# Row sums two steps earlier, four score buffers, and bias and head copies moved between engines

## What is computed

```python
# attention: each query sees the 8 first keys and the last 96
scores = scale * q @ k.T + (-slope[h] * dist)      # masked outside the window
scores = scores - max(scores)
a = exp(scores)
a = a / (sum(a) + 1e-9)
x = a @ v                                          # (1536, 512)
# first feed forward, 512 -> 2048 -> 512
h = x @ w_in
g = (a0 + a1*h + a2*h**2 + a3*h**3) / (1 + |b0|*|h| + |b1|*h**2 + 1e-6)
x = g @ w_out
# second, 512 -> 1024 -> 512
h = x @ w2_in
s = h * softmax(h)
out = layer_norm(s) * g_ln @ w2_out
```

## Time and profile before

| | |
|---|---|
| median of 3 runs | 487.11 us (486.02 to 490.15) |
| the profiled execution | 483.23 us, of which its span 481.2 us |
| PE busy | 469.0 us (97%) |
| DVE busy | 377.9 us (79%) |
| ACT busy | 271.3 us (56%) |
| POOL busy | 55.8 us (12%) |
| granted TensorE clock | 1.00 throughout |

### The profile page before, as it was taken

One profiled execution on the slowest core, in us unless ns is written; L12 is line 12 of the kernel. 1 busy time (PEld: TensorE's weight loads), 2 busy tenths in 40 slices (PEclk: granted clock), 3 DMA queues, 4 the chain that ended last, 5 costly groups with the idle time before them and its releaser, 6 DMA issues.

```text
span 481.2 us, 7546 instructions
## 1 busy us (share of the span) xinstructions
PE 469.0 (97%) x2734; PEld 383.1 (80%) x2734; DVE 377.9 (79%) x705; ACT 271.3 (56%) x481; POOL 55.8 (12%) x123
## 2 busy tenths in 40 slices
PE   7889999999999999999999999999999999999997
PEld 5667778888888878888888788888888888888885
DVE  6989989999999989877889999999685555555550
ACT  6989998656656465455555545543454333333341
POOL 4868770000000000000000000000000000000000
PEclk9999999999999999999999999999999999999999
DMA  8897964000000000000033445331012222222201
GB/s 296 295 384 268 350 252 178 1 0 1 0 1 1 0 1 0 1 1 0 1 93 105 131 140 158 113 93 44 1 44 67 66 65 65 65 68 78 72 23 44
DMA packets 25665, 42.91 MB, mean 89 GB/s; under 512 B 2080, under 2 KB 16800, under 8 KB 24480
## 3 DMA queue, kind: packets, MB, share of 16 engines
q1 hardware_dynamic: 23760, 36.64, 22.2%
q0 software_dynamic: 1296, 5.24, 3.7%
q10 hardware_dynamic: 576, 0.60, 0.4%
HBM read 33.04 MB, written 3.15 MB: 75 GB/s over the span
## 4 chain that ended last, share of the span: by engine, by line
PE 85%; ACT 7%; DMA 3%; DVE 3%; POOL 1%; issue 1%; SPq 0%; ACTq 0%; DVEq 0%
PE ps L1198 9%; PE ps L1199 9%; PE ps L1200 9%; PE ps L1129 8%; PE ps L1130 8%; PE ps L1131 8%; ACT probs L481 5%; PE ps L1263 5%; PE ps L1261 5%; PE ps L1218 5%; PE ps L1262 5%; PE ps L1217 5%; PE ps L1216 5%; PE ps L1244 2%; DMA bank_a_raw<-in_w_in 2%; PE ps L1095 2%
## 5 line engine op out<-in xcount | busy, mean ns | idle before, releaser
L1198 PE MATMUL ps<-gate_hi,bank_b_hi 128*128 128x512 f32 x192 | 74.9, 390 | 0.5 <-DVE tok_lo L942 0.5
L1129 PE MATMUL ps<-tok_hi,bank_a_hi 128*128 128x512 f32 x192 | 75.1, 391 | 0.0
L1130 PE MATMUL ps<-tok_lo,bank_a_hi 128*128 128x512 f32 x192 | 74.7, 389 | 0.0
L1199 PE MATMUL ps<-gate_lo,bank_b_hi 128*128 128x512 f32 x192 | 74.7, 389 | 0.0
L1131 PE MATMUL ps<-tok_hi,bank_a_lo 128*128 128x512 f32 x192 | 74.7, 389 | 0.0
L1200 PE MATMUL ps<-gate_hi,bank_b_lo 128*128 128x512 f32 x192 | 74.7, 389 | 0.0
L543 ACT ACTIVATE quad<-ps 128x1024 f32<-128x1024 f32 x23 | 23.7, 1030 | 57.8 <-DVE rest L880 57.8
L481 ACT ACTIVATE probs<-negs,small 128x256 f32<-128x256 f32 (+1 forms) x96 | 46.0, 484 | 0.8 <-DVE small L726 0.7
L442 POOL TENSOR_SCALAR probs<-probs,small 128x256 f32<-128x256 f32 (+1 forms) x96 | 42.6, 465 | 15.4 <-DVE small L737 15.4
L862 DVE SCALAR_TENSOR_TENSOR quad<-quad,small,absh 128x1024 f32<-128x1024 f32 x23 | 29.5, 1281 | 18.0 <-ACT absh L546 17.8
L1198 PEld LDWEIGHTS ps<-gate_hi,bank_b_hi 128*128 128x128 f32 x192 | 36.0, 188 | 8.7 <-issue 1.2
(11 more groups left out here) (103 smaller groups left out, 948.1 us busy)
## 6 DMA issues: line engine op xcount, KB each, us to landing
v_sb<-in_v_win SPq DMA_DIRECT2D x8, 704.0 KB, 6.6
bank_a_raw<-in_w_in SPq DMA_DIRECT2D x4, 1024.0 KB, 9.0
bank_b_raw<-in_w_out SPq DMA_DIRECT2D x4, 1024.0 KB, 7.1
stage_hi<-tok_hi SPq DMA_DIRECT2D x12, 256.0 KB, 2.7
stage_lo<-tok_lo SPq DMA_DIRECT2D x12, 256.0 KB, 2.8
out_dram<-out_sb SPq DMA_DIRECT2D x12, 256.0 KB, 2.0
q_sb<-in_q_t SPq DMA_DIRECT2D x14, 192.0 KB, 5.1
k_sb<-in_k_win SPq DMA_DIRECT2D x7, 384.0 KB, 8.2
```

What stands on the lines that cost most here:

```text
L1129: pe.matmul(banks(bank, 1), bank_a_hi[:, f, ws], x_hi, start=(k == 0), stop=False)
L1130: pe.matmul(banks(bank, 1), bank_a_hi[:, f, ws], x_lo, start=False, stop=False)
L1198: pe.matmul(banks(4 + k, 1), bank_b_hi[:, f, ws], g_hi, start=first, stop=False)
L1199: pe.matmul(banks(4 + k, 1), bank_b_hi[:, f, ws], g_lo, start=False, stop=False)
```

## The change

Seven things are changed, all in the attention:

1. `SUMS_AHEAD` is 4: step n makes the sums and reciprocals of units n+4 and n+5. They also stand later in the step, behind the copy of the transposed half.
2. There are four `negs` buffers. The two new ones lie in free room and in the end of `tok_hi` and `tok_lo`, which is written last.
3. The biases of the pairs of heads 1 to 3 are made by POOL (`next_bias`), behind the units 1, 3, 5 and 7 of the twelve before, and have two buffers in turn. DVE makes only the first one (`attend_bias(h)`).
4. Four of the sixteen copies to `tok_hi`, those of m = 5, 14, 23 and 32, go from ACT to DVE (`attend_high`), in front of the low part in the steps 8, 18, 26 and 36.
5. POOL's low parts of `w_in` stand behind the units 21, 23, 33 and 35 in place of 15, 21, 27 and 33.
6. POOL issues the cast of `w_in` behind unit 7 in place of 8.
7. Two waits of PE for `heads_hi`, which the wait for `heads_lo` includes, are gone.

```diff
-    negs = [[at(f"negs{i}{h}", [P, WIN], F32, w + (2 * i + h) * KB) for h in range(2)] for i in range(2)]
+    NB_NEGS = 4
...
+    bias_odd = [at(f"bias_odd{h}", [P, NB], F32, (TOK_HI, TOK_LO)[h] + 4 * (KT * T - NB)) for h in range(2)]
+    biases = (bias, bias_odd)
...
-    AHEAD, SCORES_AHEAD, SUMS_AHEAD = 6, 8, 2
+    AHEAD, SCORES_AHEAD, SUMS_AHEAD = 6, 8, 4
...
-    POOL_IN, SPLIT_FROM, SPLIT_EVERY = 4, 15, 6
-    LOADS_AT, CAST_AT = (1, 3, 4, 5), 8
+    POOL_IN, SPLITS_AT = 4, (21, 23, 33, 35)
+    LOADS_AT, CAST_AT = (1, 3, 4, 5), 7
...
+    HIGH_ON_DVE = (5, 14, 23, 32)
...
+        def next_bias(pr, h, cols):
+            pool.tensor_scalar(biases[pr % 2][h][:, cols], dist[:, cols], small[:, SLOPE_COL + 2 * pr + h:SLOPE_COL + 2 * pr + h + 1],
+                               1.0, ALU.mult, ALU.mult).then_inc(pool_bias, 1)
+
+        BIAS_AT = {1: (0, slice(WIN, NB)), 3: (1, slice(WIN, NB)), 5: (0, slice(0, WIN)), 7: (1, slice(0, WIN))}
...
-                f, part = divmod(n - SPLIT_FROM, SPLIT_EVERY)
-                if part == 0 and 0 <= f < POOL_IN:
-                    split_in_low(f)
+                if n % NPB in BIAS_AT and n // NPB + 1 < PAIRS:
+                    next_bias(n // NPB + 1, *BIAS_AT[n % NPB])
+                if n in SPLITS_AT:
+                    split_in_low(SPLITS_AT.index(n))
...
             for m in outs_at(n):
-                attend_out(m)
+                if m not in HIGH_ON_DVE:
+                    attend_out(m)
...
-            if h == 0 and n >= 2:
-                dve.wait_ge(exp_ready, 2 * (n - 1))
+            if h == 0 and n >= NB_NEGS:
+                dve.wait_ge(exp_ready, 2 * (n - NB_NEGS + 1))
...
+        def attend_high(n):
...
+            dve.wait_ge(values_ready, n + 1)
+            dve.tensor_copy(tok_hi[:].rearrange("p k t -> p (k t)")[:, bass.ds(pr * T + (b * S + half * HALF), HALF)],
+                            banks(6 + half, 1, HALF)).then_inc(high_dve, 1)
...
-            if n + SUMS_AHEAD < HEADS:
-                attend_sums(n + SUMS_AHEAD)
             if k < HEADS:
                 if pr and m == 0:
-                    dve.wait_ge(bias_ready, 4 * pr)
+                    dve.wait_ge(pool_bias, 4 * pr - 2)
                 attend_shift(k, 0)
-                if pr and m == 0:
-                    dve.wait_ge(shifted_ready, 2 * k)
-                    attend_bias(pr, 0, OF_WINDOW)
-            if n + SUMS_AHEAD < HEADS:
-                attend_reciprocals(n + SUMS_AHEAD)
             if k < HEADS:
                 attend_shift(k, 1)
...
             attend_copy(n)
...
+            if n + SUMS_AHEAD < HEADS:
+                attend_sums(n + SUMS_AHEAD)
             if k < HEADS:
-                for h in range(2):
-                    attend_shift(k + 1, h)
-            if k < HEADS and m == BLOCKS + 2 and pr + 1 < PAIRS:
-                for h in range(2):
-                    attend_bias(pr + 1, h, OF_FIRST)
+                if pr and m == 0:
+                    dve.wait_ge(pool_bias, 4 * pr)
+                attend_shift(k + 1, 0)
+            if n + SUMS_AHEAD < HEADS:
+                attend_reciprocals(n + SUMS_AHEAD)
+            if k < HEADS:
+                attend_shift(k + 1, 1)
```

More of the change, by code:

```diff
@@ L87, in attention_feed_forwards @@
     PB, TB = 8, 4
-    negs = [[at(f"negs{i}{h}", [P, WIN], F32, w + (2 * i + h) * KB) for h in range(2)] for i in range(2)]
+    NB_NEGS = 4
+    own_negs = 4 * (KT * T - (S // 2) - WIN)
+    negs_at = [w + j * KB for j in range(4)] + [w + (20 + j) * KB for j in range(2)] + [TOK_HI + own_negs, TOK_LO + own_negs]
+    negs = [[at(f"negs{i}{h}", [P, WIN], F32, negs_at[2 * i + h]) for h in range(2)] for i in range(NB_NEGS)]
     w += 4 * KB
@@ L118, in attention_feed_forwards @@
     cols(H - 1)
-    negmax = [cols(2) for _ in range(2)]
+    negmax = [cols(2) for _ in range(NB_NEGS)]
     psums = [cols(4) for _ in range(PB // 2)]
@@ L124, in attention_feed_forwards @@
     var_bias = cols()
-    unused = [cols() for _ in range(5)]
+    unused = [cols() for _ in range(3)]
     q_base, q_nmax, q_sum, q_eps, q_rec, q_max = cols(), cols(), cols(), cols(), cols(), cols()
@@ L256, in outs_at, with highs_on_act @@
             [m for m in (DONE_B0 - 1,) if n == HEADS - 4]
+    HIGH_ON_DVE = (5, 14, 23, 32)
+    def highs_on_act(n):
+        return len([m for m in range(2, n + 1, 3) if m not in HIGH_ON_DVE])
     def windowed(eng):
@@ L702, in _, with attend_bias @@
         dve.wait_ge(dve_const, made[0])
[L704 to L710, removed]
+        def attend_bias(h):
+            dve.tensor_scalar(bias[h][:, WIN:NB], dist[:, WIN:NB], slope8[:, h:h + 1], 0.0, ALU.mult, ALU.add,
+                              accum_out=unused[h]).then_inc(bias_ready, 1)
         def attend_shift(n, h):
-            par, i = n % 2, n % BLOCKS
+            buf, i = n % NB_NEGS, n % BLOCKS
             if h == 0 and n < 4:
@@ L721, in attend_shift @@
             lo = 0 if i else P
-            if h == 0 and n >= 2:
-                dve.wait_ge(exp_ready, 2 * (n - 1))
+            if h == 0 and n >= NB_NEGS:
+                dve.wait_ge(exp_ready, 2 * (n - NB_NEGS + 1))
             src = scores_of(n, h)[:, lo:WIN]
-            bs = bias[h][:, 0:WIN] if i else bias[h][:, WIN:NB]
-            dve.tensor_tensor_reduce(negs[par][h][:, lo:WIN], src, bs, -SCALE, 3.0e38, ALU.add, ALU.min,
-                                     negmax[par][:, h:h + 1]).then_inc(shifted_ready, 1)
+            own = biases[n // NPB % 2][h]
+            bs = own[:, 0:WIN] if i else own[:, WIN:NB]
+            dve.tensor_tensor_reduce(negs[buf][h][:, lo:WIN], src, bs, -SCALE, 3.0e38, ALU.add, ALU.min,
+                                     negmax[buf][:, h:h + 1]).then_inc(shifted_ready, 1)
         def attend_sums(n):
@@ L897, in _ @@
         for h in range(2):
-            attend_bias(0, h, OF_FIRST)
+            attend_bias(h)
         dve.wait_ge(bias_ready, 2)
@@ L1190, in down @@
                 if f == 0:
-                    pe.wait_ge(heads_hi, HEADS)
                     pe.wait_ge(heads_lo, HEADS)
```

32 lines of the change are left out of this document (18 added, 14 removed).

## The result

The changed kernel takes 480.78 us (median of six runs, 480.60 to 481.08). The kernel before, on the same chip, takes 486.56 (median of six, 484.33 to 490.15). The ratio is 0.9879, with a 95% interval of 0.9852 to 0.9906: faster by 1.2%, or 5.8 us. The forecast was 484.2 us with a gain of 2.9, within 1% of before. Profile against profile it is another matter: 483.23 us before, 480.79 after, a gain of 2.44, close to the 2.9 of the sum.

A forecast was written before the change was run, and what follows sets the result against it. The prediction took ACT, with DVE nearly as tight, to bound the attention and PE the feed forwards. Gap 2.14, biases 0.3 and head copies 0.5 summed to 2.9 us, set against the median 487.11: 484.2 us, range 481.0 to 487.0.

The forecast's parts named there:

- What bounds it: Attention: ACT has no idle time, DVE next to none; feed forwards are fixed PE work, so attention gains move the end equally.
- The gap: Steps 14 to 18: POOL's first low part waits 2.79 us for the raw quarter of w_in; all 2.14 us go.
- The 1.8 us that POOL was to be ahead: POOL reaches the moved first low part at 34.5 instead of 36.3, working further ahead with sums four units ahead.
- The spare of 0.7 and 0.5 us: Units 20 to 25: POOL ends units 23 and 25 at 37.65 and 40.5; PE needs them at 38.4 and 41.0.
- Rival B: The gap is larger in plain runs than in the profile: gain up to 6 us, 481; chance 0.15.
- Head copies: Four copies leave ACT, 1.48 us; DVE is late in steps 8 and 26 and two others, so 0.5 us.
- Biases: Twelve pieces move from DVE, which loses 4.9 us, to POOL at 0.46 and 0.36 us each; gain 0.3 us.
- the rule on the shared port: GpSimd shares VectorE's second port; were bias pieces to hold DVE throughout, 4.9 us, a loss of up to 2.
- Sums lead: Sums four units ahead let POOL work ahead and hide the low parts; without that cover each step loses 1.27 us.
- The cast: Cast of w_in one unit earlier only moves its bytes away from the raw quarter's; nothing taken for it.
- POOL as the bound: POOL's load for twelve units, 14.9 us against ACT's 15.2, passes it: slower, 492 us; chance 0.05.
- the wait that only moves: Raw quarter lands 3 us later than profiled, POOL still waits at unit 21: gain 0 to 1, 486.6; chance 0.06.

The follow-up runs named there:

- the third execution: The kernel before with nothing edited, profiled once more as the second of three further executions: 484.11 us.

## Why the prediction was wrong in size

**What bounds it: right.** 2.30 us gained in the attention came out at the end in full, and the feed forwards did not change.

**The gap: right in the profile.** All of it went, 14 to 20 fell to 7.61. POOL reached the first low part at 35.23 (34.5 predicted), the second at 38.31 (37.65): both 0.7 late, by its wait of 0.74 for DVE's reciprocals at 33.42, which the prediction had at 32.7. (The 1.8 us that POOL was to be ahead has no working in the prediction.) The spare of 0.7 and 0.5 us was used up, but ACT's copy of step 20 came later too, at 38.33 and not 37.8, and PE waited for POOL less than 1 us over the whole attention.

**The step that failed:** "The median of the runs shown is 487.11, 3.9 above it; I set the 2.9 against the median". That takes the 3.9 for something that the change leaves alone. Moving the low parts alone, which the prediction prices at 2.14, gave 3.6, and the cast alone, three units earlier, gave 3.8, where it takes nothing for one unit: what the median had over the profile was mostly the gap itself. By the estimate above it is a longer wait, 1.2 to 1.4 us, and the fallen clock, 1.0 to 2.3; that the clock falls there is shown by the traces, how the median's 3.3 us divides is not. Rival B named the first half and gave 481 for its far end, which is what came out; it had 0.15. It did not have the clock, so that its number fits is in part luck. The prediction says that the clock is "at its upper level there as everywhere", which was true of the profile read and of 1 of 47 runs. Set against the profiled execution alone, the same sum gives the 480.3 that the prediction states, 0.5 us from the result.

**Sum by profile:** 2.9 predicted, 2.44 measured. By ACT's copies from step 0 to 42 it took 55.76 us before, 53.44 after, and 53.14 with the head copies on ACT. So:

| term | predicted | measured |
|---|---|---|
| gap | 2.14 | 10.06 - 7.75 = 2.3 |
| biases, and what else is not head copies | 0.3 | 55.76 - 53.14 - 2.3 = 0.3 |
| head copies | 0.5 | 53.14 - 53.44 = -0.3 |

The 7.75 is 14 to 20 with the head copies on ACT.

**Head copies: mis-sized.** For step 8 DVE's times were met. The copy took 0.66 us from start to start where 0.57 was taken, and DVE began 0.06 earlier. DVE in the timeline of the changed kernel, and ACT behind it, beside the earlier trace rows:

```profile
21.39 0.69 DVE L762 COPY probs_t<-ps 128x512 f32<-128x512 f32 x1
...
22.82 0.55 DVE L769 CAST tok_hi<-ps 128x384 fp32r<-128x384 f32 x1
23.48 0.56 DVE L781 TENSOR_TENSOR tok_lo<-ps,tok_hi 128x384 fp32r<-128x384 f32 x1
23.95 0.42 DVE L743 CUSTOM_DVE_ANT_0 negs<-ps,bias_odd 128x256 f32<-128x256 f32 x1
```

```profile
24.41 0.51 ACT L499 ACTIVATE probs<-negs,small 128x256 f32<-128x256 f32 x1 [0.40 <-DVE small L743]
```

The shift was forecast at 23.95 and the exponential at 24.41, with a wait of 0.34. What was wrong is where ACT would have been without the head copy. The prediction had it there at 24.07, with its copy at 22.61. The copy stood at 22.45, and ACT was there at 22.45 + 1.46 = 23.91. Between the two starts ACT thus lost 0.50, not 0.34, and the step is 0.14 longer for the edit where 0.03 was to be won, there and at step 26. And behind steps 18 and 36 the prediction had "the whole gain stays", 0.37 each; 16 to 18 did gain 0.37, then 18 to 20 gave back 0.22 and 20 to 22 gave back 0.15. The 0.15 was predicted (0.14), the 0.22 was not: that a head copy on ACT in the next step gives DVE the time it needs did not hold.

**Biases: right from before, wrong as a price.** The pieces on POOL are near what was taken (0.46 and 0.36 us from start to start), by group and form in the changed kernel (busy us, mean ns | idle before):

```profile
L448 POOL TENSOR_SCALAR bias_odd<-dist,small 128x256 f32<-128x256 f32 x4 | 1.9, 486 | 0.0
L448 POOL TENSOR_SCALAR bias_odd<-dist,small 128x128 f32<-128x128 f32 x4 | 1.5, 380 | 0.0
```

Had they held DVE up, the gain would have been a loss; nothing of it shows, and the rule on the shared port that spoke against the change has no sign in these traces. The Trainium skill ("Advanced Engine Details and Errata", VectorE Performance Modes) has it for GpSimd's instructions beside those of VectorE that use two ports; which of VectorE's do here no row shows. Beside the head copies on ACT, where the biases and all else come to 0.3, the term held. With the head copies on DVE it is 1.4 by the steps. In the kernel before with only the low parts moved, the pieces on DVE stand beside 0.6 us lost between the steps 26 and 28, which the kernel before does not lose: what they cost depends on the gap as well.

**Sums lead: direction right, size wrong.** "without that cover each step loses 1.27" made it the edit that the low parts rest on. Undone, it cost 0.7 in all, and PE waited for POOL only 0.5 us: the cover that the prediction took for needed is mostly not.

**The cast:** "I take nothing for it" holds behind the moved low parts only. Without them the cast three units earlier is worth 3.8 us, as much as they are. One unit earlier was not run by itself.

**POOL as the bound, and the wait that only moves:** neither came. From 25 to 45 us POOL is busy for 18.14 of 20 us, 9.1 of 10 where 9.5 was forecast, and no low part waits.

## What to carry to other kernels

Compare the profiled execution with the median of the plain runs, time and mean clock of each, before making the sum: if they differ by more than the runs of a kernel without waits would, a wait in the profile is likely larger in the plain runs, and a change that removes it takes that part too. An idle stretch of PE can cost twice, once as the wait and once, where the clock falls, as PE's slower work behind it. Where two edits cure one wait, try each alone: here their gains of 3.6 and 3.8 us did not add. When work is moved onto an engine with little slack, price all moves onto it together, as what one of them costs depends on the others.

## What was unexpected of the hardware

- PE's clock fell to 0.50 behind idle times of 1.83, 2.23 and 2.88 us, and stayed at 1.00 behind 2.06; nearer the start, in two other kernels, it fell near idle times of 1.35 and 1.65. In the kernel before it stayed down for some 3 to 7 us (an estimate from the stretches of 2 us) although PE was busy for nearly all of them, and cost 1.0 to 2.3 us. The profile page's line of the clock in 40 slices shows a 9 throughout for the third execution (mean 0.996), since a slice is 12 us; stretches of 2 us show the 0.50.
- A cast of 1 MB and a load of 1 MB issued 1.2 us apart delay the load: it took 9.8 to 10.9 us from issue to use in four executions and 12.8 in a fifth, 8.6 with the cast 4 to 6 us ahead. POOL's wait was 1.33 us in place of 2.6 to 3.6.
- Between the head copy on DVE and the low part that reads it lie 0.66 us from start to start (22.82 to 23.48), against 0.47 from that low part to the shift behind it, which needs nothing of the low part (23.48 to 23.95).
